# Two row tiles for the scores, one masked pass for the maximum, squares on GpSimd, and MLP groups written out

## The reference

```python
scores = scale * q @ k.T                       # scale = 1/8
scores = where(mask[head], scores, -1e9)       # plain: 0 <= rel < 32; dilated: rel < 128 and rel % 4 == 0
attn = exp(scores - max(scores)); attn /= sum(attn) + 1e-9
x = attn @ v                                   # rows of 512: 2304 tokens
```

## Time and profile before

| | us |
|---|---|
| runs: median (lowest to highest) | 880.99 (878.39 to 881.24) |
| the profiled execution | 879.44 |
| its span, first to last instruction | 877.5 |
| TensorE busy | 823.3 (94%) |
| VectorE busy | 607.6 (69%) |
| ScalarE busy | 481.4 (55%) |
| GpSimd busy | 75.6 (9%) |
| mean granted TensorE clock | 0.978 of full speed |

### The profile page before, as it was taken

One profiled execution on the slowest core, in us unless ns is written; L12 is line 12 of the kernel. 1 busy time (PEld: TensorE's weight loads), 2 busy tenths in 40 slices (PEclk: granted clock), 3 DMA queues, 4 the chain that ended last, 5 costly groups with the idle time before them and its releaser, 6 DMA issues.

```text
span 877.5 us, 15798 instructions
## 1 busy us (share of the span) xinstructions
PE 823.3 (94%) x4902; PEld 745.4 (85%) x4902; DVE 607.6 (69%) x1169; ACT 481.4 (55%) x919; POOL 75.6 (9%) x134
## 2 busy tenths in 40 slices
PE   5999999749999999999989999999999999999993
PEld 3787876439999999999988999988999988999992
DVE  6888886575555566455567777778777788777762
ACT  3557765315545545444456666676656676656651
POOL 4022112141001000000000000001000002000002
PEclk9999999959999999999999999999999999999998
DMA  6498986234444443444242122123212214121001
GB/s 138 93 221 181 193 198 184 70 109 156 129 165 163 144 129 119 139 144 144 73 145 73 49 73 71 51 63 130 72 49 71 72 48 145 48 72 59 14 0 72
DMA packets 114911, 93.67 MB, mean 107 GB/s; under 512 B 65816, under 2 KB 94488, under 8 KB 114848
## 3 DMA queue, kind: packets, MB, share of 16 engines
q1 hardware_dynamic: 109920, 78.81, 31.1%
q0 software_dynamic: 4928, 14.16, 4.9%
HBM read 83.51 MB, written 9.44 MB: 106 GB/s over the span
## 4 chain that ended last, share of the span: by engine, by line
PE 78%; DVE 7%; DMA 5%; issue 4%; ACT 3%; POOL 1%; DVEq 0%; ACTq 0%; POOLq 0%; SPq 0%
PE bank L687 23%; PE bank L689 23%; PE bank L688 23%; DMA xtok<-x_rows 3%; PE bank L585 2%; PE bank L564 2%; PE bank L638 2%; PE bank L729 1%; PE bank L573 1%; DMA x_rows<-osb 1%; PE bank L654 1%; PE bank L548 1%; ACT yh L1010 1%; DMA dn_raw<-in_moe_w_out_dram 1%; DVE row_max L1156 1%
## 5 line engine op out<-in xcount | busy, mean ns | idle before, releaser
L687 PE MATMUL bank<-yh,up_l 128*128 128x384 f32 x384 | 129.7, 338 | 2.4 <-DVE yl L1409 2.4
L689 PE MATMUL bank<-yh,up_h 128*128 128x384 f32 x384 | 130.1, 339 | 0.0
L688 PE MATMUL bank<-yl,up_h 128*128 128x384 f32 x384 | 129.4, 337 | 0.0
L687 PE MATMUL bank<-dn_h,hid 128*128 128x512 f32 x288 | 113.0, 392 | 4.5 <-DVE hid L1431 4.2
L689 PE MATMUL bank<-dn_h,hid 128*128 128x512 f32 x288 | 113.9, 395 | 0.0
L688 PE MATMUL bank<-dn_l,hid 128*128 128x512 f32 x288 | 113.7, 395 | 0.0
L1219 DVE TENSOR_TENSOR dn_l<-dn_raw,dn_h 128x512 fp32r<-128x512 f32 (+1 forms) x80 | 71.9, 900 | 53.3 <-ACT dn_h L905 53.3
L1025 ACT ACTIVATE work<-bank 128x384 f32<-128x384 f32 x96 | 47.2, 491 | 81.4 <-PE bank L689 78.4
L687 PE MATMUL bank<-xh,up_l 128*128 128x352 f32 x256 | 85.2, 333 | 1.7 <-DVE xl L1351 1.4
L1037 ACT ACTIVATE work<-work 128x384 f32<-128x384 f32 x96 | 50.4, 525 | 66.0 <-DVE work L1426 66.0
L1421 DVE TENSOR_SCALAR work<-work 128x384 f32<-128x384 f32 x96 | 34.5, 360 | 75.3 <-ACT work L1025 75.3
(11 more groups left out here) (194 smaller groups left out, 1659.1 us busy)
## 6 DMA issues: line engine op xcount, KB each, us to landing
up_raw<-in_moe_w_dram SPq DMA_DIRECT2D x32, 512.0 KB, 3.5
dn_raw<-in_moe_w_dram SPq DMA_DIRECT2D x32, 512.0 KB, 3.4
up_raw<-in_moe_w_in_dram SPq DMA_DIRECT2D x24, 512.0 KB, 3.2
dn_raw<-in_moe_w_out_dram SPq DMA_DIRECT2D x24, 512.0 KB, 3.4
qn<-in_q_dram SPq DMA_DIRECT2D x32, 144.0 KB, 2.8
kn<-in_k_dram SPq DMA_DIRECT2D x32, 144.0 KB, 3.3
xtok<-x_rows SPq DMA_DIRECT2D x4, 1152.0 KB, 7.5
x_rows<-osb POOLq DMA_DIRECT2D x8, 288.0 KB, 3.9
```

Of the source, the lines that this page charges most:

```text
L687: mm(o, w[1], x[0], start=first, stop=False, skip_group_check=True)
L688: mm(o, w[0], x[1], start=False, stop=False, skip_group_check=True)
L689: return mm(o, w[0], x[0], start=False, stop=last, skip_group_check=True)
```

## The change

It has four parts.

1. The heads' scores become two row tiles. `kT` loses its zero columns: each head's k and q stay on their own 64 partitions. A step makes four matmuls of 64 rows and 128 columns, head 0 into bank 2 and head 1 into bank 3. Both banks belong to every step, so the scores wait for VectorE's pass of the step before. The mask matmul, its identity and the mask's casts go. `half_out` is one copy of 128 partitions. The order within a step's four blocks becomes head, then tile.
2. VectorE adds the band, scales by -1/8 and takes the minimum in one instruction for each block of 128 columns, four a step. ScalarE takes the exponential with scale -1 and that minimum as bias, four instructions a step. ScalarE's steps no longer hold squares.
3. GpSimd takes the squares of the batch before, three tiles in each of pairs 2 and 3 of a batch, behind that pair's store: a product, and then nine halvings by addition, each waiting for the one before. ScalarE keeps the last batch's six, after attention.
4. The MLP's loops on TensorE, ScalarE and VectorE are written out, three groups one after the other, without conditions. SyncE's loop stays.

```diff
-        kT = [sb2(f"kT{i}", [P, 2, WINDOW + S]) for i in range(2)]
+        kT = [sb2(f"kT{i}", [P, WINDOW + S]) for i in range(2)]
...
-                pe.wait_ge(sub_done, b * STEPS + s + 1)
-                o = bank[2 + s % 2]
-                mm(o[:QT, :], ident_bf[:], mask[:, p // 2, 2 * u:2 * u + 2, :, :].rearrange("p t h c -> p (t h c)"),
-                   start=True, stop=False, skip_group_check=True)
+                pe.wait_ge(masked_done, b * STEPS + s + 2)
                 for i in range(2):
                     t = 2 * u + i
-                    last = mm(o[:QT, i * 256:(i + 1) * 256].rearrange("p (h c) -> p h c", h=2), qT[p % 2][:, t * QT:(t + 1) * QT],
-                              kT[p % 2][:, :, t * QT:t * QT + KW], start=False, stop=True, skip_group_check=True)
+                    for h in range(2):
+                        rows = slice(h * D, (h + 1) * D)
+                        last = mm(bank[2 + h][:QT, i * KW:(i + 1) * KW], qT[p % 2][rows, t * QT:(t + 1) * QT],
+                                  kT[p % 2][rows, t * QT:t * QT + KW], start=True, stop=True, skip_group_check=True)
...
-                V.tensor_reduce(row_max[:, s % 2, :], sc, AX_X, ALU.max).then_inc(max_done, 1)
-                dve.wait_ge(max_done, G + 1)
                 dve.wait_ge(exp_done, G + 1)
-                tt(shifted[s % 2][:].rearrange("p (a c) -> p a c", a=4), sc,
-                   row_max[:, s % 2, :].unsqueeze(2).broadcast_to([QT, 4, KW]), ALU.subtract).then_inc(sub_done, 1)
+                dve.sem_inc(carrier, 1)
+                for a in range(4):
+                    h, i = divmod(a, 2)
+                    last = V.tensor_tensor_reduce(masked[s % 2][:, a * KW:(a + 1) * KW], bank[2 + h][:QT, i * KW:(i + 1) * KW],
+                                                  band[:, BANDS[p // 2][2 * u + i], :], -SCALE, 3.0e38, ALU.add, ALU.min,
+                                                  neg_max[:, s % 2, a:a + 1])
+                last.then_inc(masked_done, 1)
...
-                A(probs[s % 2][:], shifted[s % 2][:], ACT.Exp, scale=SCALE).then_inc(exp_done, 1)
+                for a in range(4):
+                    cols = slice(a * KW, (a + 1) * KW)
+                    last = A(probs[s % 2][:, cols], masked[s % 2][:, cols], ACT.Exp, scale=-1.0, bias=neg_max[:, s % 2, a:a + 1])
+                last.then_inc(exp_done, 1)
...
+            def squares(b, p):
+                last = within(b - 1, B - 2, "under b > 0") * NT
+                links = 2 * (1 + HALVINGS) + 1
+                first = b * links
+                if p == PAIRS - 2:
+                    pool.wait_ge(x_in, b * 16)
+                t = 3 * (p - PAIRS + 2)
+                done = first + (1 + HALVINGS) * (p - PAIRS + 2)
+                rows = xtok[:, bass.ds(last + t, 3), :]
+                g.tensor_tensor(pool_junk[:], rows, rows, ALU.mult).then_inc(sq_step, 1)
+                pool.wait_ge(sq_step, done + 1)
+                for h in range(HALVINGS):
+                    n = DM >> (h + 1)
+                    o = pool_ssq[:, t:t + 3].unsqueeze(2) if n == 1 else pool_junk[:, :, 0:n]
+                    g.tensor_tensor(o, pool_junk[:, :, 0:n], pool_junk[:, :, n:2 * n], ALU.add).then_inc(sq_step, 1)
+                    pool.wait_ge(sq_step, done + (h + 2))
...
-            with pe.Fori(0, NM) as m:
+            for m in range(NM):
```

More of the change, by code:

```diff
@@ L270, in before_this @@
         def before_this(eng, i, work):
+            if isinstance(i, int):
+                if i > 0:
+                    work()
+                return
             with eng.If(i > 0):
@@ L287, in half_out @@
         def half_out(copy, p, half):
[L289 to L298, removed]
+            o = kT[p % 2][:, WINDOW:WINDOW + S]
+            i = bank[half][:, 0:3 * QT]
+            if p % PAIRS < PAIRS // 2:
+                o = o[:, half * 3 * QT:(half + 1) * 3 * QT]
+            else:
+                o = o.rearrange("p (r i) -> p r i", r=DIL)[:, :, half * SEG // 2:(half + 1) * SEG // 2]
+                i = i.rearrange("p (i r) -> p r i", r=DIL)
+            last = copy(o, i)
             last.then_inc(tr_out[half], 1)
@@ L482, in _ @@
             assert steps[0] == EMB_STEPS, steps[0]
+            def squares(b, p):
[14 more added lines that the diff above has]
+                    pool.wait_ge(sq_step, done + (h + 2))
+                if p == PAIRS - 1:
+                    g.tensor_copy(ssq[:, bass.ds(last, NT)], pool_ssq[:]).then_inc(sq_step, 1)
+                    pool.wait_ge(sq_step, first + links)
+                    pool.sem_inc(carrier, 1)
             with pool.Fori(0, B) as b:
@@ L496, in _ @@
                             pool.dma_start(xr[r, i0:i0 + j1 - j0], o[j0:j1, t:t + 4:3, :]).then_inc(stored[slot], 16)
+                    if p >= PAIRS - 2:
+                        with pool.If(b > 0):
+                            squares(b, p)
             steps = [0]
@@ L818, in _ @@
                     else:
-                        with pe.If(m > 0):
+                        if m > 0:
                             mlp_up(m, i)
@@ L861, in probsT_out, with squares @@
                 A(probsT[s % 2][:], bank[4 + s % 2][:, 0:4 * QT], ACT.Copy).then_inc(pt_out, 1)
[L863 to L869, removed]
+            def squares(t):
+                act.wait_ge(x_in, B * 16)
+                act.wait_ge(ssq_done, t + 1)
+                A(sq_junk[:], xtok[:, (B - 1) * NT + t, :], ACT.Square,
+                  accum_out=ssq[:, (B - 1) * NT + t:(B - 1) * NT + t + 1]).then_inc(ssq_done, 1)
             act.wait_ge(dve_step, 1)
@@ L1071, in _ @@
             act.sem_inc(carrier, 1)
-            with act.Fori(0, NM) as m:
+            for m in range(NM):
                 for i in range(2 * FT2):
@@ L1084, in _ @@
                     else:
[L1085 removed]
+                        if m < NM - 1:
                             mlp_weights_hi(m, i)
@@ L1088, in _ @@
                     if i == 0:
-                        with act.If(m < 1):
+                        if m < 1:
                             last_block_out()
@@ L1127, in _ @@
             link(cp(band[:, 2, :], late_row[:]))
-            for kind, which in enumerate(((1, 0, 0, 0, 0, 0), (1, 2, 0, 1, 2, 0))):
-                for t, w in enumerate(which):
-                    last = cp(mask[:, kind, t, :, :], band[:, w:w + 1, :].broadcast_to([QT, 2, P]))
-            last.then_inc(init_done, 1)
             def emb_rows():
@@ L1461, in _ @@
             dve.sem_inc(carrier, 1)
-            with dve.Fori(0, NM) as m:
+            for m in range(NM):
                 for i in range(2 * FT2):
@@ L1478, in _ @@
                     if i == 0:
-                        with dve.If(m < 1):
+                        if m < 1:
                             last_block_out()
```

56 lines of the change are left out of this document (25 added, 31 removed).

## The result

The changed kernel takes 892.68 us (median of 4, 885.94 to 898.12), the kernel before in the same session 880.76 (878.39 to 881.24): ratio 1.0145, interval 1.0086 to 1.0205. It is slower, and above the predicted range. The profiled execution took 897.84 us, span 896.0, so its losses are at the upper end of that spread.

What follows compares the result with a forecast made beforehand. TensorE was taken to bound the kernel (78% of the chain), with VectorE near its limit in attention. 879.44 - 2.1 - 2.1 - 6.3 + 6.9 + 2.5 = 878.3, given as 878.5 us, range 866 to 889.

Steps and rivals of the forecast that it cites:

- Attention without GpSimd: -6.3: Attention apart from GpSimd's squares: middle batches shorten from 31.9 to 29.3 us, first and last together save 1.3; total -6.3 us.
- two signs of being wrong: In attention: GpSimd's call ends before the next store is due, or VectorE's wait for scores exceeds 1 us every step.
- Start, -2.1: Start of attention: without the mask's casts k's copy runs earlier, scores begin at 10.4 instead of 12.48; -2.1 us.
- Scores hold TensorE 0.65: Attention step on TensorE: eight half-row score instructions take 0.65 us, between 0.43 side by side and 1.1 with a changeover pause.
- rival C: Attention's scores and pass: losing the second bank decides, pairs take 8.7 us instead of 8.0, +11; 885 to 889 us; chance 0.22.
- VectorE's pass, 1.2: Attention step on VectorE: four passes of 128 columns, each delivering a minimum, take 1.2 us, between 0.92 and 1.9.
- Exponentials, 0.66 to 0.93: Attention step on ScalarE: four exponentials take 0.66 to 0.93 us where one took 0.63, hidden by free time.
- Rival D: Attention: the forecast case plus TensorE pauses costing clock, up to 1.5 us each, or written-out groups giving nothing; 881 to 884; chance 0.14.
- Squares on GpSimd, +6.9 and +2.5: GpSimd's 9.35 us calls delay stores: v late in the last two batches, +6.9 us, and the last rows late, +2.5.
- Rival B: GpSimd's squares: call under about 6.5 us or v not late, giving 869 us, range 865 to 873; chance 0.22.
- MLP, -2.1: MLP group boundaries: writing the loops out removes TensorE's 1.04 us wait at two boundaries; -2.1 us, none to -4.

Runs made afterwards that it cites:

- e7: e3 with two heads' scores in one 256-column matmul and the banks alternating by step, as before the change: 880.97 us, 1.0010 of the kernel before.
- e12: e3 without the squares of the first three batches (sums set to 1), so no GpSimd calls: 874.45 us, 0.9949 of the kernel before.
- e1: The kernel before with only the MLP's groups written out on TensorE, ScalarE and VectorE: 874.5 us against 878.22, 0.9955.
- e10: The changed kernel without the squares of the first three batches (sums set to 1), so no GpSimd calls: 872.64, 881.75, 901.05 and 911.33 us.
- e2: The changed kernel with the squares back on ScalarE, GpSimd only storing: 895.5 us, 1.0192 of the kernel before.
- e9: The changed kernel with twelve full-row fp32 matmuls on the identity around its first transposes: 891.88, 894.62, 913.06 and 918.5 us.
- e13: The changed kernel, half rows kept, with the squares shared between GpSimd and ScalarE as in e11: 876.41, 908.8, 911.97 and 914.01 us.
- e3: The changed kernel with k padded with zeros again, so scores read 128 rows, still one bank per head: 882.31 us, 1.0042 of the kernel before.
- e14: e13 with two fp32 matmuls of 128 rows and 128 columns ahead of each step's scores: 882.92 us against 878.97 for the kernel before, 1.0045.
- e6: e3 with GpSimd's two calls moved behind the stores of pair 3 and of the next batch's pair 0: 882.19 us, 1.0031 of the kernel before.
- e8: e6 and e7 together, full-row scores in alternating banks and GpSimd's calls moved: 882.91 us, 1.0042 of the kernel before.
- e11: e7 with the squares shared, three tiles a batch in one GpSimd call behind pair 3's store, three on ScalarE: 875.86 us against 878.78, 0.9946.
- e5: The changed kernel with two 96-row bf16 filler matmuls ahead of each step's scores, TensorE also waiting for GpSimd's last constants: 890.98 us, 1.0116 of the kernel before.

## Why the prediction was wrong

The step that failed is "Attention without GpSimd: -6.3", and in it the clock of TensorE, which the sum put at its full level throughout. Neither of the two signs of being wrong that the prediction gave came (the call did outlast the next store's due time, and VectorE did not wait 1 us in every step), because neither was about the clock. By its own steps, in its order:

- **Start, -2.1.** The first scores came at 10.32 (forecast 10.4), but at half pace, and the first store left at 29.47 where it left at 28.67. The step was right, and the lower level, which lasted to 40 us instead of 16, took it.
- **Scores hold TensorE 0.65.** 0.61 at full pace: right. The Trainium skill, TensorEngine Tiling (Array Packing), Key Properties, says that a change of the tiling mode drains TensorE; 0.61 leaves no room for two dear drains. So rival C was not it: e7's second bank is worth 1.3 to 2.8 us of the 11 that C asked for.
- **VectorE's pass, 1.2.** 0.93, the lower bound. The row shows the pair of instructions of which the Trainium skill speaks (VectorE: DVE Perf Modes, Two Vector instructions with no wait between them), but the second one is hidden.
- **Exponentials, 0.66 to 0.93.** 1.28: above my upper bound. One of 128 columns takes 0.39 by the page's mean and one of 512 took 0.63, so a quarter of the width is far from a quarter of the time. It is not hidden everywhere: at full pace one step of a pair waits 0.54 for the probabilities in the changed kernel (at 43.72) and 0.74 in e7.
- **Attention without GpSimd, -6.3. This step failed, and twice.** With full rows (e12 against e1) all of it is 0, and the start's 2.1 with it. With half rows at full pace, pairs are 7.13 us (7.12 to 7.34 in the changed kernel, 56 to 70 us) where 6.9 was forecast and 7.8 was before; the two middle batches in e10 took 29.8 and 30.7 us (62.02 to 91.85 to 122.52) against the 29.3 forecast and 31.9 before. So the mechanism exists, at 1.0 to 2.0 us a batch where 2.5 was forecast. But it needs TensorE at 2.4 GHz, and half rows are what made it lose that level for long: the changed kernel spent some 30 us at the start and 62 us behind the wait for v at 1.2 GHz.
- **Rival D had part of the mechanism and not the size.** I priced a pause from the earlier trace rows at up to 1.5 us, 3 us of slow matmuls. That row is of full-row matmuls, and for them it was right: e7's falls behind the waits for v last 3 to 3.5 us. With half rows a wait of 1.12 us in e2 was followed by 54 slow us, one of 3.84 in the changed kernel by 62, one of 3.82 in e9 by 10, and one of 0.73 in e10 by 3.5. I carried a recovery time from one kind of work to another; that was the fault. D also needs a pause, and e13's 131 slow us have none to blame: they begin with the first scores, and TensorE idles 1.3 us in all of them.
- **Squares on GpSimd, +6.9 and +2.5.** Forecast 9.4 together, e3 less e12 gives 7.9. Call and store came as written (9.4, 90.41). The wait for v was 3.84 us once in the changed kernel; in e3 it came twice, 4.6 us together, with 1.6 for the last rows. Rival B, the short call, was wrong.
- **MLP, -2.1.** -3.7 (e1). I had counted only the pause at each boundary, 1.04 us, where TensorE's waits for `hid` fell by 2.6 us in all; the bound of -4 holds.

The sum in measured terms: -3.7 (MLP) +7.9 (GpSimd) and about 0 (the rest of attention, full rows) is +4.2, and e3 is at +4.1 (882.31 against 878.22). From there to the changed kernel, 1.0042 to 1.0145, another 9 us: the half rows and the lower level that came with them.

What is shown: half-row against full-row scores, with nothing else changed but k's zeros and the copies that go with them, decide it (e3), with the GpSimd calls and without (e12 against e10), and full-row fp32 work in the same steps brings the level back with the half rows still there (e14). The spread says the same: all 43 executions of the six experiments with full rows and the masked pass (e3, e6, e7, e8, e11, e12) took under 885 us, and of the 20 with half rows and no filler (the changed kernel, e2, e9, e10, e13) 17 took over 885, up to 918.5. What is not shown: why. TensorE was busy in both, so the busy time of the profile alone does not tell the level; e14 adds rows and arithmetic at once, and e5's 96-row bf16 filler was not enough. How long a fall lasts is open too, and why one execution of e13 took 876.41 and three over 908.

## What to carry to other kernels

Price a matmul that uses half of the rows at both levels of the clock, and look at durations by time, not at the busy share: a TensorE that is 99% busy can be at half pace. Padding with zeros to full rows held TensorE 0.29 us longer a step here (0.90 from 103.12 to 104.02 in e3, against 0.61) and was worth 9 us. Before moving work to an idle engine's queue, compare one call with the distance of the transfers which that queue issues: 9.4 us does not fit into 7.8. Two calls a batch cost 7 to 8 us in either place (e3 and e6 against e12); one, behind a store with two pairs of room, cost nothing clear (e11). And keep the part of a change that stands alone: no kernel here was clearly faster than the one with only the MLP groups written out (e1).

## What the runs showed that I had not expected

- TensorE stayed at its 1.2 GHz level for 131 us while busy 130.4 of 131.7 (e13). The Trainium skill, TensorE: Matmul & The Clock Gate, What's actually happening, says that the clock is held down by default and set by how busy TensorE has been. Here the measurement decides: with 64-row fp32 scores in every step, being busy by the profile's count was not enough.
- The granted clock column is 1.00 in stretches before the first record of a change, whatever the level was: 1.17 us for a block that takes 0.68 at full pace. The mean of a run inherits this: e13's profiled execution, 908.8 us, has a mean granted clock of 0.98, as the kernel before has.
- The product of a tile with itself on GpSimd, 1536 elements a lane, took 2.82 us, 1.8 ns an element; I had read 2.2 ns from the earlier trace rows.
- Four exponentials of 128 columns with a bias for each partition took 1.28 us, 0.39 each by the page's mean, where one of 512 columns took 0.63.
